# MLP2 in units of 512 tokens without transposes; MLP1's weights split by GpSimd; own orders for the prologue and the first three chunks

## What is computed

```python
for t in range(S):
    new_re = ar * S_re - ai * S_im          # a, normalised to a magnitude of at most 0.999
    new_im = ar * S_im + ai * S_re
    S_re, S_im = new_re + k_t v_t^T, new_im
    y[t] = q_t @ S_re
```

## Time and profile before

| | us |
|---|---|
| median of 3 runs | 1250.98 |
| lowest, highest | 1248.17, 1251.94 |
| the profiled execution | 1250.42 |
| its span, first to last instruction | 1248.4 |
| TensorE matmuls busy | 1171.6 (94%) |
| VectorE busy | 691.9 (55%) |
| ScalarE busy | 674.3 (54%) |
| GpSimd busy | 242.0 (19%) |

### The profile page before, as it was taken

The page is one execution under the profiler, slowest core; times in us unless marked ns, Lnnn a source line. Parts: engine busy times, 40 slices in busy tenths (PEclk is TensorE's granted clock), DMA queues, the critical chain, the costliest instruction groups (busy, mean ns, idle before and its releaser), DMA issues.

```text
span 1248.4 us, 27248 instructions
## 1 busy us (share of the span) xinstructions
PE 1171.6 (94%) x11112; PEld 1117.2 (89%) x11112; DVE 691.9 (55%) x1130; ACT 674.3 (54%) x1321; POOL 242.0 (19%) x269
## 2 busy tenths in 40 slices
PE   2666999999999999999999989999999999999998
PEld 1555998999999999989989979999999999999997
DVE  4899778787787787787787402342232222222222
ACT  5777777777777777777776324522122222222221
POOL 1001333323433323333433334000000000000000
PEclk9878999999999999999999979999999999999999
DMA  4322111212111122111121022400010101010000
GB/s 141 123 91 71 39 40 59 78 48 76 39 59 58 40 59 63 48 58 59 39 59 52 26 91 76 140 20 20 19 39 1 39 1 39 1 39 19 1 20 19
DMA packets 42890, 62.71 MB, mean 50 GB/s; under 512 B 3856, under 2 KB 38544, under 8 KB 42384
## 3 DMA queue, kind: packets, MB, share of 16 engines
q1 hardware_dynamic: 42768, 60.98, 15.7%
HBM read 46.77 MB, written 14.16 MB: 49 GB/s over the span
## 4 chain that ended last, share of the span: by engine, by line
PE 68%; DVE 13%; ACT 12%; issue 5%; DMA 0%; DVEq 0%; ACTq 0%; SPq 0%
PE bank L1359 8%; PE bank L1360 8%; PE bank L1361 8%; PE bank L1378 4%; PE bank L1382 4%; PE bank L1380 4%; PE bank L1276 4%; PE bank L1278 4%; PE bank L1277 4%; PE bank L1289 3%; PE bank L1293 3%; PE bank L1291 3%; PE bank L1210 3%; ACT L517 2%; PE bank L1200 2%
## 5 line engine op out<-in xcount | busy, mean ns | idle before, releaser
L1097 DVE TENSOR_TENSOR prod<-bank,silu 128x384 f32<-128x384 f32 x96 | 53.5, 557 | 285.2 <-PE bank L1361 269.2
L475 POOL CAST ghi<-rg 128x384 fp32r<-128x384 f32 x128 | 92.2, 720 | 530.5 <-ACT rg L654 530.5
L771 ACT ACTIVATE silu<-bank 128x384 f32<-128x384 f32 x84 | 41.5, 493 | 280.9 <-PE bank L1361 280.9
L477 POOL TENSOR_TENSOR glo<-rg,ghi 128x384 fp32r<-128x384 f32 x128 | 146.0, 1141 | 10.2
L1276 PE MATMUL bank<-xhi,win_hi 128*128 128x384 f32 x384 | 134.7, 351 | 7.5 <-DVE xlo L1004 3.8
L1289 PE MATMUL bank<-ghi,wout_hi 128*128 128x384 f32 x384 | 131.3, 342 | 0.0
L1278 PE MATMUL bank<-xhi,win_lo 128*128 128x384 f32 x384 | 130.6, 340 | 0.0
L1277 PE MATMUL bank<-xlo,win_hi 128*128 128x384 f32 x384 | 130.4, 340 | 0.0
L1293 PE MATMUL bank<-ghi,wout_lo 128*128 128x384 f32 x384 | 129.0, 336 | 0.0
L1291 PE MATMUL bank<-glo,wout_hi 128*128 128x384 f32 x384 | 128.7, 335 | 0.0
L651 ACT ACTIVATE rg<-bank 128x384 f32<-128x384 f32 x128 | 62.2, 486 | 69.6 <-PE bank L1278 68.7
(11 more groups left out here) (158 smaller groups left out, 2936.5 us busy)
## 6 DMA issues: line engine op xcount, KB each, us to landing
gates_sb<-in_gates SPq DMA_DIRECT2D x48, 192.0 KB, 2.4
qk_sb<-in_qk SPq DMA_DIRECT2D x24, 384.0 KB, 3.1
v_sb<-in_v SPq DMA_DIRECT2D x24, 192.0 KB, 2.6
xT_scratch<-yT SPq DMA_DIRECT2D x48, 96.0 KB, 2.1
xin<-xT_scratch SPq DMA_DIRECT2D x8, 576.0 KB, 4.1
y1T_scratch<-y1s SPq DMA_DIRECT2D x8, 576.0 KB, 3.5
x<-y1T_scratch SPq DMA_DIRECT2D x8, 576.0 KB, 4.0
out<-o_sb SPq DMA_DIRECT2D x8, 576.0 KB, 3.0
```

Source lines behind the costliest of these rows:

```text
L477: pool.tensor_tensor(glo[:, j % GR, :], rg[:, j % 2, :], ghi[:, j % GR, :].bitcast(F32), ALU.subtract)\
```

## The change

- **MLP2** takes 6 units of 512 tokens (`UT2`). In down2, p is stationary and w_out moves, for four blocks of 128 tokens into banks 4 to 7, so the result comes out untransposed; y2T and transposes2 are gone. ScalarE (`results_even`) and VectorE (`results_odd`) copy two blocks each to o_sb at j = 1 of the next unit. The last unit is stored block by block.
- **The last MLP1 unit**: odd ups go to bank 3, and up(j) waits for the Relu of up(j-2); split_x(7) on ScalarE stands behind the Relu of unit 6's last up.
- **MLP1's weights**: `stage1` has four slots. GpSimd subtracts six of the seven low halves (and copies the high half of piece 0), from the prologue on; VectorE keeps piece 3. ScalarE copies the high halves of pieces 1 to 4 in the prologue, 5 and 6 in chunk 0. SyncE loads all from the prologue on, piece i waiting for the low half of piece i-4; the load of MLP1's first input waits for all seven.
- **Orders**: the prologue and chunks 0 to 2 (`early`) have orders of their own on SyncE, ScalarE, VectorE and TensorE. Chunks from 3 on, and where MLP1's works are placed, are as before.

The diff, cut; left out are renamings, sizes, and the dealing rewritten as a table with the same places.

```diff
+    CP2 = 4
+    UT2 = CP2 * CH
+    NU2 = TOK // UT2
...
+        NST = 4
+        s_wst = [sem(f"s_wst{i}") for i in range(NST)]
+        s_whi, s_whi_pool = sem("s_whi"), sem("s_whi_pool")
+        s_wlo, s_wlo_pool = sem("s_wlo"), sem("s_wlo_pool")
...
+        LAST_UP = WORKS.index(("up", NF1 - 1))
+        h_bank = lambda u, j: 3 if u == NM - 1 and j % 2 else 4
...
+        HIGH_ON_POOL, LOW_ON_DVE = (0,), (3,)
...
             def mlp1_load(u):
+                if u == 0:
+                    for i in range(len(PIECES1)):
+                        sp.wait_ge(*low_done(i))
...
+            def weight1(i):
+                src, hi, lo, dims = PIECES1[i]
+                if i >= NST:
+                    sp.wait_ge(*low_done(i - NST))
+                sp.dma_start(staged(stage1, i, dims), src).then_inc(s_wst[i % NST], 16)
 
             load_gates(0, 0, 1)
             sp.dma_start(sums_in[:, :], mats[:, P:]).then_inc(s_const, 16)
-            sp.dma_start(ident, mats[:, 0:P]).then_inc(s_const, 16)
-            sp.dma_start(yT[:, 0, :], masks).then_inc(s_const, 16)
             load_qk(0, 0, 1)
+            sp.dma_start(ident, mats[:, 0:P]).then_inc(s_flat, 16)
+            sp.dma_start(yT[:, 0, :], masks).then_inc(s_flat, 16)
+            weight1(0)
             load_v(0, 0, 1)
-            def weight1(i):
-                src, hi, lo, dims = PIECES1[i]
-                sp.wait_ge(s_wlo, max(i - 1, 0))
-                sp.dma_start(staged(stage1, i, dims), src).then_inc(s_wst[i % 2], 16)
-
-            weight1(0)
+            weight1(1)
             load_gates(0, 1, 2)
+            weight1(2)
+            weight1(3)
+            weight1(4)
             load_qk(0, 1, 2)
             load_v(0, 1, 2)
-            weight1(1)
-            weight1(2)
             carry_phase(1)
-
-            def unit(u, b_next, half, has_tail=True, has_head=True, has_next=True):
+            weight1(5)
+            weight1(6)
...
+            def store2_last(u):
+
+                for tb in range(CP2):
+                    sp.wait_ge(mlp2["odd" if tb % 2 else "acc"], 2 * u + tb // 2 + 1)
+                    sp.dma_start(out_view[:, u * CP2 + tb, :], o_sb[:, tb, :]).then_inc(mlp2["ost"], 16)
...
+            def weight1(i):
+                src, hi, lo, dims = PIECES1[i]
+                if i in HIGH_ON_POOL:
+                    pool.wait_ge(s_wst[i % NST], 16 * (i // NST + 1))
+                    pool.tensor_copy(hi, staged(stage1, i, dims)).then_inc(s_whi_pool, 1)
+                pool.wait_ge(*high_done(i))
+                pool.tensor_tensor(lo, staged(stage1, i, dims), hi.bitcast(F32), ALU.subtract).then_inc(s_wlo_pool, 1)
...
+            for i in range(len(PIECES1)):
+                if i not in LOW_ON_DVE:
+                    weight1(i)
...
+            def early(c):
+                n = c + 1
+                if c in LOAD_AT:
+                    split_x(LOAD_AT[c])
+                high_gates(n + 1)
+                works(c, (0,))
+                inverse(n + 1)
+                signs(n + 1)
+                works(c, (1, 2))
+                decays(n + 1)
+                block_decays(n + 1)
+                works(c, (3,))
+                angle(n + 1)
+                high_theta(n + 1)
+                if c == 0:
+                    weight1(5)
+                works(c, (4,))
+                if c == 0:
+                    weight1(6)
+                works(c, (5,))
+                copy32(n)
+                copy64(n)
+                squares(n + 2)
+                sines(n + 1)
+                evac_y(n)
+                magnitudes(n + 2)
+                works(c, (6,))
+                evac_Q(n + 1)
+                works(c, (7, 8, 9, 10))
+                evac_K(n + 1)
+                evac_D(n + 1)
...
             inverse(1)
+            signs(1)
             decays(1)
-            act.wait_ge(s_init, 8)
-            block_decays(1)
-            signs(1)
             angle(1)
             high_theta(1)
+            weight1(1)
             sines(1)
+            weight1(2)
             squares(2)
-            magnitudes(2)
+            exp_table()
+            block_decays(1)
+            weight1(3)
+            magnitudes(2, first=True)
             evac_Q(1)
             evac_K(1)
             evac_D(1)
-            unit(0, False, False)
-            act.wait_ge(s_wlo, len(PIECES1))
-            unit(1, False)
+            weight1(4)
+            for c in range(CPU):
...
-            for kind, j in WORKS[HEAD:]:
-                work_at(kind, j, NU - 2)
-            split_x(NU - 1)
+            for i in range(HEAD, len(WORKS)):
+                work_at(*WORKS[i], NM - 2)
+                if i == LAST_UP:
+                    split_x(NM - 1)
...
+            def results_even(u):
+                act.wait_ge(mlp2["ost"], 16 * u)
+                for tb in range(0, CP2, 2):
+                    act.wait_ge(mlp2["out"], CP2 * (NF2 * (u + 1) - 1) + tb + 1)
+                    act.activation(o_sb[:, tb, :], banks[4 + tb][:, 0:DM], ACT.Copy).then_inc(mlp2["acc"], 1)
...
+            def early(c):
+                n = c + 1
+                capped(n + 1)
+                log_gates(n + 1)
+                denominator(n + 1)
+                to_borders8(n)
+                if c == 0:
+                    clear_state(0, c)
+                if c in LOAD_AT:
+                    split_x(LOAD_AT[c])
+                low_gates(n + 1)
+                to_borders16(n)
+                to_borders32(n)
+                in_block(n)
+                ratio(n + 1)
+                to_borders64_Q(n)
+                neighbours8(n)
+                phases(n + 1)
+                to_borders64_K(n)
+                low_theta(n + 1)
+                neighbours16(n)
+                to_start(n)
+                wrap(n + 1)
+                scale_qk(n + 1)
+                msq(n + 2)
+                k_end(n + 1)
+                rotate(n + 1)
+                decay_state(n)
+                state(n)
+                rotate_end(n + 1)
...
+            msq(1)
+            dve.wait_ge(s_flat, 32)
+            dve.tensor_copy(masks_sb[:, :], yT[:, 0, :]).then_inc(s_masks, 1)
+            capped(1)
+            dve.wait_ge(s_const, 16)
             dve.tensor_copy(sums_r[:, :], sums_in[:, :]).then_inc(ev["r32"], 1)
-            msq(1)
-            capped(1)
             denominator(1)
             log_gates(1)
             low_gates(1)
-
-            dve.tensor_copy(masks_sb[:, :], yT[:, 0, :]).then_inc(s_masks, 1)
-            dve.wait_ge(s_masks, 1)
             ratio(1)
-            dve.wait_ge(s_init, 8)
             phases(1)
             low_theta(1)
+            k_end(1)
+            dve.wait_ge(s_masks, 1)
             wrap(1)
+            dve.wait_ge(s_init, 9)
             scale_qk(1)
-            k_end(1)
             rotate(1)
+            msq(2)
+            weight1(3)
             rotate_end(1)
-            msq(2)
-            unit(0, False, False)
-            unit(1, False)
+            for c in range(CPU):
+                early(c)
...
+            def results_odd(u):
                 dve.wait_ge(mlp2["ost"], 16 * u)
-                for tb in range(CPU):
-                    dve.wait_ge(mlp2["tr"], CPU * u + tb + 1)
-                    dve.tensor_copy(o_sb[:, tb, :], banks[2 + tb][:, 0:DM]).then_inc(mlp2["otr"], 1)
+                for tb in range(1, CP2, 2):
+                    dve.wait_ge(mlp2["out"], CP2 * (NF2 * (u + 1) - 1) + tb + 1)
+                    dve.tensor_copy(o_sb[:, tb, :], banks[4 + tb][:, 0:DM]).then_inc(mlp2["odd"], 1)
...
-                pe.wait_ge(mlp1["act"], base + j)
+                pe.wait_ge(mlp1["act"], base + j - (1 if u == NM - 1 and j else 0))
...
+            def early(c):
+                n = c + 1
+                scores_mid(n)
+                scores8(n)
+                gate_sums(n + 1)
+                works(c, (0, 1, 2))
+                block_sums(n + 1)
+                works(c, (3, 4, 5, 6, 7))
+                scores16(n)
+                scores32(n)
+                works(c, (8,))
+                scores64(n)
+                works(c, (9,))
+                phase_sums(n + 1)
+                outputs(n, 0)
+                transposes_Q(n + 1)
+                works(c, (10,))
+                state(n)
+                transposes_K(n + 1)
...
             def down2(u, j):
 
-                pe.wait_ge(mlp2["acc"], KT3 * u)
+                pe.wait_ge(mlp2["acc"], 2 * u)
+                pe.wait_ge(mlp2["odd"], 2 * u)
                 pe.wait_ge(mlp2["lo"], u * NF2 + j + 1)
-                for m in range(KT3):
-                    c, dst = slice(m * P, (m + 1) * P), banks[5 + m][:, 0:UT]
-                    nc.tensor.matmul(dst, wo_hi[:, j, c], p_hi[:, j % GR, :], start=j == 0, stop=False,
+                for tb in range(CP2):
+                    t, dst = slice(tb * CH, (tb + 1) * CH), banks[4 + tb][:, 0:DM]
```

(16 more changed lines are left out.)

341 lines of the change are left out of this document (164 added, 177 removed).

## The result

| | before | after |
|---|---|---|
| median, us | 1250.47 (4 runs) | 1237.45 (4 runs, 1235.34 to 1239.05) |
| ratio of the runs | | 0.9906, 95% interval 0.9886 to 0.9926 |
| span of the profiled execution, us | 1248.4 | 1233.5 |

What follows compares the result with a forecast made beforehand. VectorE was taken to bound the first three chunks, TensorE nearly all the rest. Against 1250.42 us, -10.7 (seam), -12.7 (MLP2), -3.5 (end) and -3 (front) sum to -29.9, giving 1220.5 us, range 1204 to 1233.

Steps and rivals of the forecast that it cites:

- Part 1, the seam: Last MLP1 unit: earlier split_x(7) closes TensorE's gap, clock stays up, 49.9 us replace 60.6: -10.7 us.
- Rival (d): Last MLP1 unit: the gap stays open, the clock falls, about 8 us come back: 1228.5 us; chance 0.06.
- Part 2, MLP2: MLP2 in units of 512 tokens: fewer up matmuls at a fixed 13.3 ns, no y2T transposes: -12.7 us.
- rival (b): MLP2: the 13.3 ns are a share of the columns, 0.231 us a matmul, total 1226.3 us; chance 0.12.
- (e): MLP2: 0.173 is a floor under each matmul, 512 columns take 0.213 us, total 1203 us; chance 0.04.
- Part 3, the end: After the last matmul: one copy, its issue and a 192 KB store, 3.4 us instead of 6.9: -3.5 us.
- Part 4, the front: Prologue and chunks 0 to 2: low halves move to GpSimd, -18 + 15 = -3 us net, bounds -18 and +10.
- Rival (a): Front: GpSimd's long instructions hold VectorE no longer than short ones, -18 us there, total 1205.5 us; chance 0.22.
- (c): Front: GpSimd's holds of VectorE cost nearly their whole length, total 1230 to 1233 us; chance 0.09.
- The first: Prologue: phases(1) can start near 14.8, so chunk 0's border products start at 29.8 instead of 32.8 if GpSimd costs nothing.
- The second: Chunks 0 to 2: without VectorE's low halves a chunk takes 24.2 - 3.5 = 20.7, say 21.0 us.
- Rival (f): Chunk 3: the last low half comes late and SyncE's waiting load stops all, slower than before; chance 0.02.

Runs made afterwards that it cites:

- The two exchanges: Changed kernel with MLP2's gate and value in each other's PSUM bank, then with each other's weights, both from the second unit on: 1236.82 and 1237.93 us.
- the fastest kernel: Changed kernel with the front of before, but a lean prologue: piece 0's high half on GpSimd, its low half on VectorE, no high halves on ScalarE; 1221.35 us.

## Why the prediction was wrong

**Part 1, the seam: right.** -10.7 forecast, -10.6 measured, -10.9 alone. The gap closed, the clock stayed up, and 288 matmuls took 49.99 us. Rival (d) fell.

**Part 2, MLP2: right in its mechanism, one term too large.** The fixed 13.3 ns hold: 0.2267 us in the value's pass is the forecast to the last digit, and rival (b) with 0.231 and (e) with 0.213 fall there. The N/2.4 + 2.5 ns of the Trainium skill (TensorE: Matmul & The Clock Gate, Back-to-back issue gap) would be 0.2158 us for 512 columns; the page gives it for an isolated matmul, and the trace doesn't show it in any of these passes. The step that failed is that all passes would go at that pace: a step was to take 6.16 us and takes 6.23, the gate's pass 0.04 more and the down products 0.03 more (0.176 us each on average where they were 0.173 when p moved and the weights were stationary, though the last six of a step keep that pace). 72 such steps are the 4.7 us that are missing, within the rounding. The two exchanges show that the gate's share goes with the place in the step; its cause, and that of the down products', stays open.

**Part 3, the end: right**, 3.0 us from the last matmul's end where 3.4 were forecast.

**Part 4, the front: wrong, and it carries most of the miss.** The profiled execution (1235.34) lies 14.8 us over the forecast, which was made against the profiled execution of before; 11.2 are the front's and 4.7 MLP2's, and the attention, the seam and the end together give 0.8 back. The prediction put together -18 if GpSimd costs nothing, and +15 for its holds. Against the kernel whose GpSimd only fills:

| term | forecast | measured |
|---|---|---|
| holds | +15 (20 less 5) | +13.0 (20.2 less 7) |
| prologue without holds | -3.0 | -0.6 |
| chunk 0 without low halves | 29.8 to 21.0 | 29.8 to 26.3 |
| chunk 1 | 24.3 to 21.0 | 24.3 to 23.2 |
| chunk 2 | 24.2 to 21.0 | 24.2 to 24.5 |
| all without holds | -18 | -4.8 |

The hold, which was called the likeliest error, was the best of the estimates: where it would fall, for how long, and nearly how much of it would be covered. That the two sums of 20.2 agree to the digit is luck: the subtractions were shorter (4.5 and 3.4 us, not 4.9 and 3.7), and in chunk 0 the first operation held was not a two-input one but the scaling of St. That a long GpSimd instruction holds two-input VectorE ones to its end, as the Trainium skill has it (SBUF — State Buffer, Who interferes with whom), is in the rows of 14.39 to 30.5 us above. The 4.5 us of the Trainium skill for an addition of two inputs of 2048 elements (GPSIMD Engine Reference, Elementwise — side-by-side cycle accounting) is what the trace shows for the subtraction, where the prediction scaled up to 4.9. Rival (a), no long holds, fell; so did (c), since 7 of the 20 us were covered by other waiting.

Two steps failed. The first: "in the new order it can start near 14.8. So if GpSimd costs nothing, chunk 0's border products start at 29.8". phases(1) does start at 14.39, but the prediction counted GpSimd's and VectorE's share of the moved weights and left out ScalarE's: the high halves of pieces 1 to 3, 1.89 + 1.89 + 1.47 = 5.25 us, now stand in ScalarE's row of the prologue, and two of them, 3.36 us, on its chain. Without them the border product starts at 29.72, the forecast's number (that kernel also loads the weights later and has no fills, but no step of the chain with fills waits for either). A part that is moved takes all its instructions along, on every engine.

The second: "a chunk takes 24.2 - 3.5 = 20.7, say 21.0". It was read from VectorE's busy share, 23.30 of 24.26 us, that each low half taken away would shorten the chunk by its length. With both gone VectorE idles 1.9 us ahead of L1057 in chunk 1, for the state's matmuls, while TensorE and ScalarE carry the chain outputs, copy of y, table load, logarithms, copies of Q, K and D. The prediction named ScalarE's chain as about as long as 21.0 us, but gave TensorE's part in it no time, and that part ran at the lower clock: 3.4 us for the outputs. So the chunk takes 23.1 us at a clock of 0.78, 22.9 at 0.85, and 23.9 to 25.5 in other executions and orders at lower ones, 24.0 on average, next to the 24.2 with two low halves. At the upper clock the outputs would be 1.7 us shorter and the chunk near 21.4, an estimate from the distances of 0.43 and 0.22 us; no run shows it. An engine that is busy for 96% of a stage bounds it only until the chain beside it does, and that chain was 1 us away or less.

For chunk 0 the same 21.0 stood in the sum although the prediction's own loss of 6.8 us leaves 29.75 - 6.8 = 23.0: 2 of the 18 us were never worked out. It measured 26.3 with a fill. In that trace the fill holds the scaling of St by 1.2 us, and ScalarE's high halves of pieces 5 and 6 (43.74 to 46.58) stand ahead of its copies of AT, which VectorE had ready at 45.37, 1.1 us: the first failed step again.

**Rival (f)** didn't come: nothing waited for the last low half.

The range missed by two errors of the same sign. The front's +8.2 lies within part 4's own bounds of -18 and +10 and alone gives 1220.5 + 11.2 = 1231.7, inside the range; MLP2's 4.7 carries it to 1236.4, beyond the 1233 at which the range ended, since it allowed for the worst front and nothing beside it.

## What to carry over

Before a low-cost engine is given a two-input job, ask who else reads SBUF at that moment: here 12.1 us of VectorE's work became 24.5 us on GpSimd, and the price on the critical path rose from about 9 to about 13 us. Cut into short instructions the job costs 7.5, but in the fastest kernel it stood on VectorE, one piece in its waiting time and two a chunk. And what a stage gains from a lighter engine is bounded by the next chain in it: find that one, by the idle time that the freed engine would have and at the clock that its TensorE part gets, before subtracting durations.

## What the runs showed of the chip

- A VectorE operation with a single SBUF input, the scaling of St with a factor a partition (L1066), is held as well: 3.67 us beside GpSimd's subtraction, 0.42 alone. Beside a fill by GpSimd (1.80 us for 2048 elements) VectorE's two-input operations kept their 0.55 us, but this one took 1.59 and ended 0.21 behind the fill of 1.38 us, so it isn't the two reads alone that hold it.
- The hold ends with the GpSimd instruction under way, and the VectorE operation then goes ahead of the next one: 0.53 us with pieces of 256 elements, 4.31 us with one of 2048.
- A matmul of fp32r with 128 stationary columns takes 13.3 ns over its columns at 2.4 GHz, at 384 (0.1733 us) as at 512 (0.2267), and in a first pass behind other products 0.231.
- A stage of the same work took 24.9 us at a granted clock of 1.00 and 29.0 at 0.76, and a chunk with the same instructions up to its end 23.1 at 0.78 and 24.5 at 0.65. More matmuls in the stage ahead raised the clock there and in the one traced execution did not keep it up in the next.
- A low granted clock costs nothing while another engine bounds the stage (chunk 2 with two low halves on VectorE: 24.2 us at 0.72 and at 1.00), and begins to cost when that engine is relieved.
